# A rational gate on VectorE: the quotient as a high and a low half, with GpSimd summing the denominator

## The reference

```python
# N = 6016 tokens, C = 256, F = 2048
qn = q / (norm(q, axis=1) + 1e-6);  kn = k / (norm(k, axis=1) + 1e-6)
s = kn.T @ qn / tau                     # 256 x 256
a = exp(s - s.max(-1));  a /= a.sum(-1) + 1e-9
x = v @ a                               # N x 256
# first feed-forward: a rational gate
h = x @ w_in                            # N x 2048
P = a[0] + a[1]*h + a[2]*h**2 + a[3]*h**3
Q = 1 + abs(b[0])*abs(h) + abs(b[1])*h**2
y = (P / (Q + 1e-6)) @ w_out            # N x 256
# second feed-forward: the other gate
h = y @ w_in2
out = (h * clip(h + 3, 0, 6) / 6) @ w_out2
```

## Time and profile before

| | before |
|---|---|
| median of 3 runs | 1240.01 us |
| lowest and highest run | 1239.97 and 1242.56 us |
| span of the profiled execution | 1240.4 us |
| its own time beside the span | not listed apart from the span |
| PE busy | 1165.5 us (94%), 5440 matmuls |
| DVE busy | 1156.9 us (93%), 1723 instructions |
| ACT busy | 961.1 us (77%), 1782 instructions |
| POOL busy | 360.6 us (29%), 276 instructions |

### The profile page before, as it was taken

The page is one execution under the profiler, slowest core; times in us unless marked ns, Lnnn a source line. Parts: engine busy times, 40 slices in busy tenths (PEclk is TensorE's granted clock), DMA queues, the critical chain, the costliest instruction groups (busy, mean ns, idle before and its releaser), DMA issues.

```text
span 1240.4 us, 17387 instructions
## 1 busy us (share of the span) xinstructions
PE 1165.5 (94%) x5440; PEld 954.5 (77%) x5440; DVE 1156.9 (93%) x1723; ACT 961.1 (77%) x1782; POOL 360.6 (29%) x276
## 2 busy tenths in 40 slices
PE   7876788899999999999999999999999999999998
PEld 6755566787787787787787787787787787888898
DVE  5779999999999999999999999999999999999872
ACT  6566787888887887887887887887887887787864
POOL 2146576222222222222222222222222222222334
PEclk9887899999999999999999999999999999999999
DMA  9730000000000000000000000000000000000000
GB/s 319 265 111 1 18 1 1 1 26 1 1 34 1 0 34 0 0 34 0 0 34 0 0 34 0 0 34 0 0 34 1 1 31 1 1 26 1 18 1 22
DMA packets 16210, 33.65 MB, mean 27 GB/s; under 512 B 1824, under 2 KB 6176, under 8 KB 15904
## 3 DMA queue, kind: packets, MB, share of 16 engines
q1 hardware_dynamic: 16160, 33.04, 7.5%
HBM read 26.87 MB, written 6.16 MB: 27 GB/s over the span
## 4 chain that ended last, share of the span: by engine, by line
PE 41%; DVE 37%; issue 18%; ACT 3%; DMA 0%; DVEq 0%; SPq 0%; POOL 0%; ACTq 0%
DVE T L771 7%; PE H L334 6%; DVE G L784 6%; DVE T L750 6%; PE H L336 6%; PE H L335 6%; DVE SQ L764 5%; DVE R L798 5%; DVE g_lo L792 4%; PE OP L343 3%; PE OP L334 3%; PE OP L336 3%; PE OP L335 3%; PE YP L334 3%; PE YP L336 3%
## 5 line engine op out<-in xcount | busy, mean ns | idle before, releaser
L307 POOL TENSOR_TENSOR g_lo<-R,g_hi 128x512 fp32r<-128x512 f32 (+2 forms) x208 | 267.1, 1285 | 754.9 <-ACT g_hi L598 754.9
L563 ACT ACTIVATE T<-H,coef 128x512 f32<-128x512 f32 (+2 forms) x208 | 153.0, 735 | 161.0 <-PE H L336 160.9
L777 DVE SCALAR_TENSOR_TENSOR Y<-SQ,Y 128x512 f32<-128x512 f32 (+2 forms) x208 | 206.0, 991 | 0.5
L334 PE MATMUL H<-vT_hi,wf_hi 128*128 128x512 f32 (+2 forms) x416 | 159.8, 384 | 20.6 <-DVE T L756 15.2
L334 PE MATMUL H<-yT_hi,wu_hi 128*128 128x512 f32 (+2 forms) x416 | 157.7, 379 | 11.2 <-DVE R L798 10.5
L764 DVE TENSOR_TENSOR SQ<-SQ,AB 128x512 f32<-128x512 f32 (+2 forms) x192 | 167.4, 872 | 0.0
L334 PE MATMUL YP<-g_hi,wd_hi 128*128 128x512 f32 (+2 forms) x416 | 160.0, 385 | 6.3 <-DVE yT_lo L804 5.6
L771 DVE SCALAR_TENSOR_TENSOR T<-T,coef,Y 128x512 f32<-128x512 f32 (+2 forms) x208 | 163.0, 784 | 0.0
L334 PE MATMUL OP<-g_hi,wd_hi 128*128 128x512 f32 (+2 forms) x416 | 156.8, 377 | 1.8 <-ACT o_tok L621 1.5
L336 PE MATMUL YP<-g_hi,wd_lo 128*128 128x512 f32 (+2 forms) x416 | 157.0, 377 | 0.0
L335 PE MATMUL YP<-g_lo,wd_hi 128*128 128x512 f32 (+2 forms) x416 | 156.9, 377 | 0.0
(11 more groups left out here) (89 smaller groups left out, 2259.6 us busy)
## 6 DMA issues: line engine op xcount, KB each, us to landing
qk<-in_q SPq DMA_DIRECT2D x23, 256.0 KB, 5.6
qk<-in_k SPq DMA_DIRECT2D x23, 256.0 KB, 7.0
v_raw<-in_v SPq DMA_DIRECT2D x10, 512.0 KB, 3.6
out<-o_tok SPq DMA_DIRECT2D x10, 512.0 KB, 3.7
w_raw_b<-in_moe_w_out SPq DMA_DIRECT2D x8, 512.0 KB, 5.7
w_raw_a<-in_moe_w_in SPq DMA_DIRECT2D x1, 2048.0 KB, 11.5
w_raw_b<-in_moe_w_in SPq DMA_DIRECT2D x4, 512.0 KB, 6.1
v_raw<-in_v SPq DMA_DIRECT2D x2, 256.0 KB, 7.1
```

The costliest lines, as they stand in the source:

```text
L307: nc.gpsimd.tensor_tensor(g2_lo[:, j % 4, 0:w], R[:, j % 4, 0:w], g2_hi[:, j % 4, 0:w].bitcast(fp32), ALU.subtract).then_inc(g2_lo_done, 1)
L334: nc.tensor.matmul(psum, w_hi, x_hi, start=first, stop=False)
L563: nc.scalar.activation(T[:, j % 4, 0:w], H1[:, j % 2, 0:w], ACT.Identity, bias=A2, scale=A3)
L777: nc.vector.scalar_tensor_tensor(Y[:, j % 2, 0:w], SQ[:, j % 4, 0:w], Q_CONST, Y[:, j % 2, 0:w], ALU.add, ALU.mult).then_inc(e_done, 1)
```

## The change

VectorE now forms g1_hi directly, rounded as it is written, and gets the low half from the remainder: g1_hi = round((T+a0)*Y), SQ = (SQ+Q0)*g1_hi, T = (T+a0)-SQ, g1_lo = T*Y. These are four instructions, each reading what the one before it wrote. The Newton step, the tile G and ScalarE's rounding copy `a3` are gone. GpSimd makes the sum SQ+AB in every block, ahead of `g2_split` in its list, and no longer makes g1_lo in blocks 0 and 1. The lags become 2 (LAG_DIVIDE), 4 (LAG_DOWN1, was 5) and with it SHIFT2 5 (was 6). VectorE's order in a slot becomes horner_2, horner_1, gate2, the four of the quotient. In the fresh slot TensorE's order is up2, transpose, down2, up1, down1, where it was up2, transpose, down2, down1, up1.

```diff
-    LAG_NEWTON = 2
-    LAG_SPLIT1 = 3
-    LAG_DOWN1 = 5
+    LAG_DIVIDE = 2
+    LAG_DOWN1 = 4
...
             def step(t):
                 for j in range(J):
+                    if exists(t):
+                        q_body(t, j)
...
-                    if isinstance(t, int) and t in POOL_SUMS:
-                        q_body(t, j)
-                    x = stage(t, j - LAG_SPLIT1)
-                    if x and isinstance(x[0], int) and x[0] < POOL_SPLITS:
-                        g1_split(*x)
                     if x := stage(t - 1, j - SHIFT2 - 1):
                         g2_split(*x)
...
+                        up1(t, j)
                         if d1:
                             down1(*d1)
-                        up1(t, j)
...
-                wait_chunk(act, g1_done, back(t, j, 4))
+                wait_chunk(act, g1_lo_done, back(t, j, 4))
                 nc.scalar.activation(T[:, j % 4, 0:w], H1[:, j % 2, 0:w], ACT.Identity, bias=A2, scale=A3)
-                wait_chunk(act, e_done, back(t, j, 4))
...
-                wait_chunk(act, g1_done, back(blk, j, 2))
+                wait_chunk(act, g1_lo_done, back(blk, j, 2))
                 nc.scalar.activation(Y[:, j % 2, 0:w], SQ[:, j % 4, 0:w], ACT.Abs_reciprocal_sqrt, bias=Q_CONST)\
...
-            def a3(blk, j):
-                w = width(blk)
-                wait_chunk(act, g1_done, (blk, j))
-                wait_chunk(act, d1_done, back(blk, j, 4))
-                nc.scalar.activation(g1_hi[:, j % 4, 0:w], G[:, j % 2, 0:w], ACT.Copy).then_inc(g1_hi_done, 1)
...
+            def quotient_hi(blk, j):
+
                 w = width(blk)
                 wait_chunk(dve, y2_done, (blk, j))
                 wait_chunk(dve, t3_done, (blk, j))
+                wait_chunk(dve, d1_done, back(blk, j, 4))
+                nc.vector.scalar_tensor_tensor(g1_hi[:, j % 4, 0:w], T[:, j % 4, 0:w], A0, Y[:, j % 2, 0:w],
+                                               ALU.add, ALU.mult).then_inc(g1_hi_done, 1)
+
+            def product(blk, j):
+
                 w = width(blk)
                 wait_chunk(dve, g1_hi_done, (blk, j))
+                nc.vector.scalar_tensor_tensor(SQ[:, j % 4, 0:w], SQ[:, j % 4, 0:w], Q_CONST,
+                                               g1_hi[:, j % 4, 0:w].bitcast(fp32),
+                                               ALU.add, ALU.mult).then_inc(product_done, 1)
+
+            def rest(blk, j):
+
+                w = width(blk)
+                wait_chunk(dve, product_done, (blk, j))
+                nc.vector.scalar_tensor_tensor(T[:, j % 4, 0:w], T[:, j % 4, 0:w], A0, SQ[:, j % 4, 0:w],
+                                               ALU.add, ALU.subtract).then_inc(rest_done, 1)
+
+            def quotient_lo(blk, j):
+
+                w = width(blk)
+                wait_chunk(dve, rest_done, (blk, j))
+                nc.vector.tensor_tensor(g1_lo[:, j % 4, 0:w], T[:, j % 4, 0:w], Y[:, j % 2, 0:w], ALU.mult)\
+                  .then_inc(g1_lo_done, 1)
...
+                    if exists(t) and not fresh:
+                        horner_2(t, j)
+                        horner_1(t, j)
+                    if u2:
                         gate2(*u2)
+                    if x:
+                        quotient_hi(*x)
+                        product(*x)
                     if j == LAG_DOWN1 - 1 and exists(t - 1):
                         yT_split(t - 1)
...
+                    if x:
+                        rest(*x)
+                        quotient_lo(*x)
                     if j == J - 1 and exists(t) and exists(t + 1):
                         vT_split(t + 1)
...
+                    if exists(t) and fresh:
+                        horner_2(t, j)
+                        horner_1(t, j)
```

More of the change, by code:

```diff
@@ L44, in attention_ffn_ffn @@
     assert N % P == 0 and C == 2 * P and J == 16 and inner >= 4
-    POOL_SPLITS = 2
     LAG_ROOT = 1
-    LAG_NEWTON = 2
-    LAG_SPLIT1 = 3
-    LAG_DOWN1 = 5
+    LAG_DIVIDE = 2
+    LAG_DOWN1 = 4
     SHIFT2 = LAG_DOWN1 + 1
     LAG_DOWN2 = 3
-    POOL_SUMS = 1,
     W0_LOADS = 8, 12, 16, 20
@@ L124, in attention_ffn_ffn @@
         T = sb("T", [P, 4, W], fp32)
-        G = sb("G", [P, 2, W], fp32)
         SQ = sb("SQ", [P, 4, W], fp32)
@@ L156, in attention_ffn_ffn @@
             sem, ("u1_done", "a1_done", "w_done", "t2_done", "t3_done", "y_done", "y2_done"))
-        s_done, e_done, g1_done, g1_hi_done, g1_lo_done, d1_done = map(
-            sem, ("s_done", "e_done", "g1_done", "g1_hi_done", "g1_lo_done", "d1_done"))
+        g1_hi_done, product_done, rest_done, g1_lo_done, d1_done = map(
+            sem, ("g1_hi_done", "product_done", "rest_done", "g1_lo_done", "d1_done"))
         u2_done, r_done, g2_done, g2_hi_done, g2_lo_done, d2_done = map(
@@ L292, in q_body @@
                 wait_chunk(pool, a1_done, (t, j))
-                if j == 0:
-                    wait_chunk(pool, w_done, back(t, 0, 1))
                 nc.gpsimd.tensor_tensor(SQ[:, j % 4, 0:w], SQ[:, j % 4, 0:w], AB[:, j % 2, 0:w], ALU.add)\
                   .then_inc(w_done, 1)
-            def g1_split(blk, j):
-                w = width(blk)
-                wait_chunk(pool, g1_hi_done, (blk, j))
-                nc.gpsimd.tensor_tensor(g1_lo[:, j % 4, 0:w], G[:, j % 2, 0:w], g1_hi[:, j % 4, 0:w].bitcast(fp32),
-                                        ALU.subtract).then_inc(g1_lo_done, 1)
             def g2_split(blk, j):
@@ L646, in step @@
                         root_squared(*x)
-                    if x := stage(t, j - LAG_SPLIT1):
-                        a3(*x)
                     if j == OT_SLOT and exists(t - 2):
@@ L815, in step @@
                             weight_hi(2, j - W_SLOTS[1])
[L816 to L819, removed]
+                    x = stage(t, j - LAG_DIVIDE)
+                    u2 = stage(t - 1, j - SHIFT2)
                     fresh = j == 0 and exists(t - 1)
[L821 to L831, removed]
+                    if exists(t) and not fresh:
+                        horner_2(t, j)
+                        horner_1(t, j)
+                    if u2:
                         gate2(*u2)
+                    if x:
+                        quotient_hi(*x)
+                        product(*x)
                     if j == LAG_DOWN1 - 1 and exists(t - 1):
                         yT_split(t - 1)
[L835 to L838, removed]
+                    if x:
+                        rest(*x)
+                        quotient_lo(*x)
                     if j == J - 1 and exists(t) and exists(t + 1):
                         vT_split(t + 1)
[L841 to L847, removed]
+                    if exists(t) and fresh:
+                        horner_2(t, j)
+                        horner_1(t, j)
             every_step(dve, step)
```

## The result

The changed kernel takes 1342.83 us (median of 4 runs, 1341.96 to 1344.82), the kernel before 1241.14 us beside it: a ratio of 1.0817, 95% interval 1.0796 to 1.0839. It is slower by 102 us, 8%. The forecast was 1323.5, its range 1258 to 1350, the main case's own range 1300 to 1345.

The account below looks back on a forecast made before the run. PE set the pace at 5.60 us a slot. Nine wide blocks 64, block 1 6, narrow blocks 15, end -1.5: +83.5 on 1240.4 gives 1323.9, median 1323.5 us, range 1258 to 1350.

Parts of the forecast that it names:

- the main case: The forecast itself: VectorE runs away behind GpSimd's lock in each block; 1323.5 us, own range 1300 to 1345, chance 58%.
- The lock: VectorE instructions with two SBUF inputs cannot run while GpSimd holds 1.17 us; lagging slot 4.87 + 0.54 + 0.98 = 6.39 us.
- Rival 3: VectorE's write-then-read pairs cost nothing extra, slot 4.39 us, no runaway; 1248 us, chance 4%.
- The trap and its spring: GpSimd's early sum keeps VectorE behind; sprung at slot 8 after out_copy's late T, quotient_lo issued 0.31 us too late.
- The yT_lo slot: Slot with yT_lo in a block: expected to pass without springing the runaway, with 0.17 us to spare.
- A wide block: Each of blocks 2 to 10: 100.4 us against 93.3, +7.1, in all 64 us.
- rival 4: Worse: PE's border waits halve its clock, 1.7 us a block; yT_lo slot may spring the trap, 1.2 more; 1350 us, 12%.
- The blocks at the ends: Block 1 at +6 us; narrower blocks 0, 11 and 12 at 5 each, 15; the end -1.5.
- The border: Block border in TensorE's fresh slot: down1, no longer done before up1, costs 1.4 us a block.
- PE under 90% in the second half of a block, full in the first: Listed sign that the forecast is right: TensorE's busy share within a block.
- rival 1: No runaway: VectorE keeps up at 5.60 us a slot, only the border costs; 1262 us, chance 18%.
- rival 2: Faster: horner_1 second in the slot removes PE's 1.51 us wait at each border; 1225 us, chance 8%.

Follow-up runs that it names:

- Experiment 1: Changed kernel with one more wait: GpSimd's sum of a chunk also waits for the low half three chunks back; 1271.51 us, ratio 1.0231.
- experiment 2: Changed kernel with ScalarE's out_copy moved behind the T, SQ and AB of the next slot; 1299.44 us, ratio 1.0455.
- experiment 8: As cited, for the lag back at 5 (sixth in the study's list): changed kernel with LAG_DOWN1 5, SHIFT2 6; 1344.29 us, ratio 1.0825.
- Experiment 9: Changed kernel, VectorE's order kept, with the added wait on GpSimd's sum and down1 ahead of up1 in the fresh slot; 1241.01 us, ratio 0.9997.
- experiment 5: Changed kernel with only TensorE's order in the fresh slot put back, down1 ahead of up1; 1318.26 us, ratio 1.0615.
- experiment 4: Changed kernel with VectorE's order interleaved: quotient_hi, horner_2, product, horner_1, rest, gate2, quotient_lo; 1250.01 us, ratio 1.0068.
- Experiment 10: Changed kernel with VectorE's order interleaved, down1 ahead of up1 in the fresh slot, and the added wait on GpSimd's sum; 1223.15 us, ratio 0.9849.

## Why the prediction was right, and where it was off

*The lock* (right). Seven VectorE instructions without lock waits were put at 4.87 us (the seven steps add up to 4.86), and the slot of a lagging VectorE at 6.39. It measured 6.32, with the two waits where they were placed, on quotient_hi and on rest (at most 0.07 us off). That dependent instructions step by 0.12 more is confirmed: 603.58 to 604.29 us and its like, 0.71 to 0.78. Rival 3, by which this costs nothing, is out, and the rule of the Trainium skill in VectorE: DVE Perf Modes (The DRAIN you can't avoid), measured there on a chain of tensor_copy, is not borne out by this kernel's pairs: a reader behind its writer starts 0.03 to 0.04 us after the writer's end, an independent instruction 0.08 before it.

*The trap and its spring* (right in the steady part). The slot behind out_copy was to miss by 0.31 us; it missed by 0.20 and lasted 6.55 against 6.5 forecast. Experiment 1 shows that the place of the holds is the cause, experiment 2 that out_copy springs it there. The yT_lo slot passed, as worked out: it took 6.34 us and the three behind it 5.41.

*A wide block*, +7.1: measured 7.7. The trace shows blocks of 100.0 us with one stretch of 3.4 us at half clock, which lies between the border's two long waits, and of 101.6 to 102.0 with two or three. The forecast of 100.4 held no clock at all. The clock is rival 4's part of the price, worth 1.0 us a block (mean 101.0) over the 100.0, where rival 4 had 1.7; its other part, a runaway from the yT_lo slot, did not come.

*The blocks at the ends* were the mis-sized term. Block 2 was counted among the wide ones with 7.1 and cost 13.7. Of what this is above the others' 7.7, 3.1 lies in the changed kernel (104.17 us against their 101.03): the forecast counted 5.60 for every slot up to the seventh, but T's 4.9 us apart spring the trap two slots earlier there, as experiment 2 shows. The other 2.8 lies in the kernel before, which took only 90.5 us for this block instead of 93.3, and the forecast left that out.

The narrow blocks were taken at 5 each, between 0 and 7.1. The last T's show the tail:

```profile
1188.58 0.57 ACT L563 ACTIVATE T<-H,coef 128x256 f32<-128x256 f32 x1 [0.49 <-PE H L336]
```

before, and after the change:

```profile
1290.11 0.55 ACT L548 ACTIVATE T<-H,coef 128x256 f32<-128x256 f32 x1
```

From there to the span's end it is 51.8 us before and 50.0 after, so the end did gain its 1.5 us (1.8; 52.5 with the lag back at 5, experiment 8). Counted from each block's first T to the next block's, block 0 cost 10.0, outside its bounds, block 11 6.7 and block 12 5.7 up to its last T; block 0's first T came 2.7 us earlier. With 64 put as 53.8 + 13.7 + 6.8 = 74.3 for the nine wide ones, 5.1 for block 1 (forecast 6) and 20.3 + 0.2 for the rest (forecast 15 - 1.5), the sum is 99.9 against 83.5 forecast; the spans differ by 99.7. Nearly every miss is to the same side, so the total did not land in its range because errors cancelled; but it is 19 us over the forecast and only 2 under the upper end of the main case's range.

*The border* (right, and worth more than its price). down1 behind up1 was put at 1.4 us a block; put back alone it gave 25 us in all and 2.1 in a wide block (15.0 us over seven), since it also leaves less time at the half clock. Experiment 9 gives 30 us for it on top of experiment 1, 2.8 a wide block, for a like reason.

*PE under 90% in the second half of a block, full in the first*: right in sum. In the block from 632 to 732 us:

```profile
632.00:682.00 50.00, 50.00 (x217) 40.07 (x216) 43.19 (x57) 36.10 (x62) 23.89 (x18) 0.98 0.06 21
682.00:732.00 50.00, 43.72 (x183) 33.64 (x182) 48.92 (x57) 31.28 (x55) 19.07 (x15) 0.97 0.00 0
```

That is 50.00 of 50 us and 43.72 of 50, 87%. But the idle time isn't spread over the slow slots: TensorE still had 12.00 us busy of 12 from 688 to 700. VectorE's lag eats slack first, and TensorE stands only from 713 us on, in four waits.

*Rivals 1 and 2* are out for the changed kernel, but rival 1's 1262 is near what experiment 1 made of it (1271). Rival 1's own sum has a sign wrong: up1 could start 0.1 us later than before, so it is +1.4 + 0.1 a block, and 1264.

## What to carry to other kernels

Where two engines share a lock, its load says little; what counts is which instruction of the other engine each hold meets, and whether being late makes that better or worse. Before moving an instruction, work out the slot once with the engines in step and once with the busy one behind: if the second is longer than the pace of the whole, one late or one early input can tip it, and a wait that looks superfluous can be worth 5%. Keep instructions that need the lock apart by ones that don't; that also hides the step from writer to reader.

## What the runs showed of the hardware

- The lock is exclusive and first come, first served for whole instructions. One GpSimd sum of 128x512 holds it for about 1.17 us (1.30 us long in the trace), and a VectorE instruction that meets it takes up to 1.82 us instead of 0.69. GpSimd gets it between two VectorE instructions even if these stand 0.04 us apart (rest ended at 683.81 + 0.75, quotient_lo was issued at 684.60, and the sum that had come at 684.40 went first). The Trainium skill (GPSIMD Engine Reference, Key points) names the contention; the runs give its size.
- TensorE's granted clock fell to half, 1.2 GHz, for stretches of 3.4 us at the borders of every wide block of the changed kernel (waits of 2.8 to 2.9 us, others before and behind them) and of experiment 1 (2.5 to 2.8). It fell at none of the wide blocks before (1.51), of experiment 4 (1.4), or of experiment 9 (1.15). With waits of 2.42 to 2.46 us in experiment 2 it fell at four of eight borders, so the length of the wait alone doesn't decide it. A stretch behind the border's last wait cost 1.3 to 1.6 us of a block (95.0 or 96.5 us in experiment 2, 98.7 or 100.2 in experiment 5, 100.0 or 101.6 in the changed kernel); one between two waits cost nothing that shows.
- Not settled: how much of experiment 4's 93 us is the shorter chain and how much the place of the holds, since one order changed both. Experiments 9 and 10 bound what the order still gives once the wait has placed the holds: 18 us.
